# Attention and two feed-forward layers on one core: one transfer of 70 long rows for the windows of values in place of six

## What is computed

```python
q_d = q.reshape(B, H, Sd, factor, D).mean(axis=3)        # factor = 4; k_d, v_d likewise
out_d = sm_attn(q_d, k_d, v_d)                           # softmax attention over 144 means
out_up = np.repeat(out_d, factor, axis=2)
mask = np.abs(pos[:, None] - pos[None, :]) < factor      # 7 positions wide
out_local = softmax(where(mask, scale * q @ k.T, -1e9)) @ v
x = (out_up + out_local).transpose(0, 2, 1, 3).reshape(B * S, H * D)     # 2304 x 512
x = elu(x @ w_in0) @ w_out0                              # 512 -> 2048 -> 512
out = (s * relu(x @ w_in1) ** 2 + b) @ w_out1
```

## Time and profile before

| | us |
|---|---|
| median of 3 runs | 888.83 |
| lowest, highest | 888.66, 889.57 |
| the profiled execution | 886.9 |
| its span | 885.1 |
| PE busy in the span | 853.1 (96%) |
| DVE busy | 621.1 (70%) |
| ACT busy | 448.7 (51%) |
| POOL busy | 66.7 (8%) |

### The profile page before, as it was taken

One profiled execution on the slowest core, in us unless ns is written; L12 is line 12 of the kernel. 1 busy time (PEld: TensorE's weight loads), 2 busy tenths in 40 slices (PEclk: granted clock), 3 DMA queues, 4 the chain that ended last, 5 costly groups with the idle time before them and its releaser, 6 DMA issues.

```text
span 885.1 us, 14880 instructions
## 1 busy us (share of the span) xinstructions
PE 853.1 (96%) x5660; PEld 777.0 (88%) x5660; DVE 621.1 (70%) x976; ACT 448.7 (51%) x928; POOL 66.7 (8%) x84
## 2 busy tenths in 40 slices
PE   5999789999999999999999999999999999999997
PEld 4888789999989999999999889989889898898995
DVE  6999887787776666755658886887756558555553
ACT  7999976545655344453435543535433235332322
POOL 5556510000000000000000000000000000000000
PEclk9999999999999999999999999999999999999999
DMA  8789925645525434353352654636645344553411
GB/s 193 189 185 201 207 63 193 213 155 190 213 91 218 168 128 170 131 185 136 129 194 74 211 178 163 207 131 228 211 143 190 131 138 171 190 189 133 138 52 72
DMA packets 44192, 143.94 MB, mean 163 GB/s; under 512 B 5120, under 2 KB 15200, under 8 KB 44128
## 3 DMA queue, kind: packets, MB, share of 16 engines
q1 hardware_dynamic: 44128, 143.07, 49.7%
HBM read 108.97 MB, written 34.08 MB: 162 GB/s over the span
## 4 chain that ended last, share of the span: by engine, by line
PE 84%; DVE 5%; ACT 3%; issue 3%; POOL 2%; DMA 2%; SPq 1%; DVEq 0%; POOLq 0%; ACTq 0%
PE ps_h L600 36%; PE ps_y L636 22%; PE ps_y L629 21%; DMA qbd<-in_qt 2%; PE ps_h L549 1%; PE ps_s L472 1%; ACT prob L669 1%; POOL v L438 1%; POOL q_half L431 1%; DVE hsum L1103 1%; PE ps_xd L525 1%; PE ps_t L496 1%; DVE prob L923 1%; DVE xs_lo L974 1%; PE ps_sd L481 1%
## 5 line engine op out<-in xcount | busy, mean ns | idle before, releaser
L1103 DVE TENSOR_TENSOR hsum<-hsum,ps_h 128x384 f32<-128x384 f32 x322 | 176.9, 551 | 167.0 <-PE ps_h L600 164.3
L600 PE MATMUL ps_h<-xs_hi,wc_hi 128*128 128x384 f32 x644 | 218.8, 340 | 1.8 <-DVE hsum L1103 1.6
L600 PE MATMUL ps_h<-xs_lo,wc_hi 128*128 128x384 f32 x644 | 217.4, 338 | 0.0
L600 PE MATMUL ps_h<-xs_hi,wc_lo 128*128 128x384 f32 x644 | 217.3, 337 | 0.0
L820 ACT ACTIVATE act_out<-act_out,sb 128x768 f32<-128x768 f32 x48 | 49.5, 1031 | 228.6 <-DVE act_out L1118 228.6
L600 PEld LDWEIGHTS ps_h<-xs_hi,wc_hi 128*128 128x128 f32 x644 | 121.0, 188 | 12.2 <-issue 1.5
L600 PEld LDWEIGHTS ps_h<-xs_lo,wc_hi 128*128 128x128 f32 x644 | 121.0, 188 | 8.8
L1124 DVE TENSOR_TENSOR g_lo<-act_out,g_hi 128x768 fp32r<-128x768 f32 x96 | 91.5, 954 | 49.6 <-ACT g_hi L831 49.6
L600 PEld LDWEIGHTS ps_h<-xs_hi,wc_lo 128*128 128x128 f32 x644 | 121.0, 188 | 0.0
L636 PE MATMUL ps_y<-wo_hi,g_hi 128*128 128x512 f32 x288 | 113.0, 392 | 1.5 <-ACT xsum L841 1.5
L636 PE MATMUL ps_y<-wo_hi,g_lo 128*128 128x512 f32 x288 | 113.9, 395 | 0.0
(11 more groups left out here) (89 smaller groups left out, 1089.7 us busy)
## 6 DMA issues: line engine op xcount, KB each, us to landing
wc_hi<-wc_kept SPq DMA_DIRECT2D x30, 896.0 KB, 4.5
wc_lo<-wc_kept SPq DMA_DIRECT2D x30, 896.0 KB, 6.4
wstage<-in_w_out SPq DMA_DIRECT2D x48, 512.0 KB, 3.6
wc_kept<-wc_hi SPq DMA_DIRECT2D x16, 896.0 KB, 3.6
wc_kept<-wc_lo SPq DMA_DIRECT2D x16, 896.0 KB, 6.3
wstage<-in_w_in SPq DMA_DIRECT2D x18, 512.0 KB, 7.1
kall<-in_kt SPq DMA_DIRECT2D x16, 288.0 KB, 4.5
qbd<-in_qt SPq DMA_DIRECT2D x32, 144.0 KB, 4.4
```

Source lines behind the costliest of these rows:

```text
L600: mm = pe.matmul(o, wc[a][:, sl % 2, W_SLOT[k], c * P:(c + 1) * P], xs[x][:, X_SLOT[k], c, :], start=(c == 0 and q == 0), stop=(c == 1 and ...
L1103: dve.tensor_tensor(part(sl, *out_at), part(sl, *in_at), ps_h[:, prod_number(sl, pos) % 2, 0:TH], op).then_inc(h_added, 1)
```

## The change

The host lays out the values a second time: for each pair 70 rows, and in row r the r-th position of all nine windows side by side, 9 x 128 numbers, 4608 bytes. `load_v` fills `vwin` with one DMA of those 70 rows. `v4` is loaded as before from the old layout. With two DMAs for each pair, NV is 2 in place of 7.

```diff
-def attention_moe_moe2(nc, q_t, k_t, v, w_in0, w_out0, w_in1, w_out1, s, b, out):
+def attention_moe_moe2(nc, q_t, k_t, v, v_t, w_in0, w_out0, w_in1, w_out1, s, b, out):
...
-    NV = 7
+    NV = 2
...
             def load_v(bb, slot):
                 vp = v[bb, slot]
-                inner = vp[QT - REACH:QT - REACH + (NT - 2) * QT].rearrange("(t r) x -> r t x", r=QT)
-                rest = vp[2 * QT - REACH:2 * QT - REACH + (NT - 2) * QT].rearrange("(t r) x -> r t x", r=QT)
-                dst = vwin[:, slot].rearrange("p t h d -> p t (h d)")
-                sp.dma_start(dst[0:QT, 1:NT - 1, :], inner).then_inc(v_loaded[slot], 16)
-                sp.dma_start(dst[QT:WIN, 1:NT - 1, :], rest[0:2 * REACH]).then_inc(v_loaded[slot], 16)
-                for t in (0, NT - 1):
-                    a = WSTART[t]
-                    sp.dma_start(dst[0:QT, t, :], vp[a:a + QT]).then_inc(v_loaded[slot], 16)
-                    sp.dma_start(dst[QT:WIN, t, :], vp[a + QT:a + WIN]).then_inc(v_loaded[slot], 16)
+                sp.dma_start(vwin[:, slot].rearrange("p t h d -> p (t h d)"), v_t[bb, slot]).then_inc(v_loaded[slot], 16)
                 sp.dma_start(v4[:, slot].rearrange("p k i x -> p k (i x)"),
                              vp.rearrange("(k p i) x -> p k (i x)", k=2, i=POOL)
                              ).then_inc(v_loaded[slot], 16)
...
+    def lay_v_tiles(x):
+
+        tiles = [x[:, :, a:a + 70] for a in [min(max(t * 64 - 3, 0), x.shape[2] - 70) for t in range(x.shape[2] // 64)]]
+        y = np.stack(tiles, axis=3)
+        return np.ascontiguousarray(y).reshape(*y.shape[:3], -1)
...
-        "in_v": np.ascontiguousarray(v.reshape(v.shape[0], v.shape[1] // 2, 2, *v.shape[2:]).transpose(0, 1, 3, 2, 4)).reshape(
-            v.shape[0], v.shape[1] // 2, v.shape[2], 2 * v.shape[3]),
+        "in_v": pairs_of_v,
+        "in_v_tiles": lay_v_tiles(pairs_of_v),
```

More of the change, by code:

```diff
@@ L1229, in lay_w_out @@
         return np.ascontiguousarray(x.transpose(2, 0, 1, 3)).reshape(128, w.shape[0] // 256, 2 * w.shape[1])
+    def lay_v_tiles(x):
+        tiles = [x[:, :, a:a + 70] for a in [min(max(t * 64 - 3, 0), x.shape[2] - 70) for t in range(x.shape[2] // 64)]]
+        y = np.stack(tiles, axis=3)
+        return np.ascontiguousarray(y).reshape(*y.shape[:3], -1)
     nc = bacc.Bacc("TRN2", target_bir_lowering=False, num_devices=1)
+    pairs_of_v = np.ascontiguousarray(v.reshape(v.shape[0], v.shape[1] // 2, 2, *v.shape[2:]).transpose(0, 1, 3, 2, 4)).reshape(
+        v.shape[0], v.shape[1] // 2, v.shape[2], 2 * v.shape[3])
     arrays = {
```

## The result

| | before | after |
|---|---|---|
| median of 9 runs each, us | 889.57 | 894.61 |
| lowest, highest | 886.87, 891.56 | 887.08, 896.70 |
| the profiled execution, us | 886.9 | 891.17 |
| its span | 885.1 | 889.4 |

The ratio is 1.0044, with a 95% interval of 1.0026 to 1.0063: slower by 5 us in the median, where I had forecast no difference that can be told and a time of 888.4 in a range that ended at 889.8. (The two medians alone give 1.0057.) The executions scatter more than before, and the fastest of them, 887.08 us, lies inside the range of the forecast. Something happens in most executions, not in all.

The account below looks back on a forecast made before the run. PE fills 84% of the chain; the change could act only in the attention stage, through SP's late issue and the DMA backlog delaying POOL twice. The sum, -0.41 us, took the median 888.83 to 888.4, range 886.7 to 889.8.

Parts of the forecast that it names:

- (1): SP's queue: 3.29 us of issue go, one of 0.4 comes; a step falls from 5.27 to 2.4 us, SP waits for values.
- (3): POOL at pair 14, attention stage: without the wait for q's DMA it starts 0.27 us earlier, and PE and ACT follow.
- (4): POOL at pair 15: starts 1.32 us earlier, but PE gains only 0.59 and ACT keeps 0.41 us.
- (6): Pace in the loop: POOL's first addition takes 1.15 us at any DMA share, so less traffic gains zero.
- D: Rival: POOL's late starts come from the backlog of weights, k and q alone and stay; 888.8 us, chance 0.10.
- (2): DMA engines: same bytes in 70 longer rows; a pair costs 4.8 to 7.0 us now and no more afterwards.
- C: Rival, much faster: short rows disturb compute or the fetching of code, so pairs speed up; 2.8 us, 886.0, chance 0.08.
- B: Rival, slower: seventy rows spread badly, SP queues everything, DMA sets the pace; pair 15's q 3.3 us later, 892.1, chance 0.08.

## Why the prediction was wrong

**Right.** Point (1) in its mechanics: 0.33 to 0.37 us for the new issue (I took 0.4), 2.4 us for a step, SP waiting for values, pair 15's q issued at 77.7 us (I said about 79). Points (3) and (4) for POOL: its late starts on a DMA went. Point (6): 1.15 us for the addition, as before. D falls with these. Whether (4)'s 0.41 us are there can't be told; the kernel held back, which has the short issue of (1), POOL in time as in (3) and (4), and no standing queue, lies at 0.9989 and 1.0009.

**The step that failed** is in (1) and (2): "Nothing of this is on the path by itself, it only makes (1) safe". I had the capacity of the DMA engines between 172 and 251 GB/s and leaned on the upper end, from a share of 0.76 at 191 GB/s; my own 4.8 to 7.0 us for a pair reached past the 6.1 us of compute, and I wrote "under or about". But a share counts the time of packets, and this grows with the queue: 200 GB/s came at 0.93 with SP ahead and at 0.76 with it held. Kept full, the engines of the three profiles of the changed kernel gave 186 to 217 GB/s in the stretches of 12 us between 28 and 88 us, and 192 to 196 with short rows. A pair is 1.207 MB, so some 6.0 us at 200 GB/s, against 6.1 us of compute: next to nothing left to drain what the head had piled up. So my forecast for the profile, k landing near 4 us, was wrong by 10 us; the share from 76 to 100 us did fall, but only to 0.93 and 0.96; and PE's first big product, forecast at 112.3 us, came at 116.16. I had priced what SP's lateness costs (POOL's two starts) and not what it gave: a queue that drained between steps. The six short issues were a brake, 3.29 us long in each step.

**What was missing** is a third reader of the DMA engines. I asked of POOL alone what it waits for, and left out PE's code, which nobody waits for by a semaphore. It stood in the page, 42 packets of q8, and a look at when these came against the places in the unrolled steps where PE needs them would have shown margins of 4 to 6 us. C had "the fetching of code" in it, with the sign turned round.

**B** had the sign right and the mechanism wrong. It put the price into q coming late because 70 rows spread badly. In the three profiles of the changed kernel q was never late after the head, and with 630 short rows the loss is the same (1.0054 against 1.0065). Late q from full engines did show in two kernels that run ahead with the long rows, in the profile with three batches in the loop and in one held in the unrolled steps alone, so B's full engines were right, and how much of the loss in other executions they make this way stays open. The rule of the Trainium skill that I set beside it, DMA: Bandwidth & Descriptors, "Why a DMA increments its semaphore by 16 and not by 1", may hold for the split over engines; no run here shows single engines, and it explains nothing of the loss. Two other places of that page bear on what happened. "Rules for kernel authors" advises to issue a DMA early and to wait for it late; here that was the harm, 5 us, as the engines were full. And "Queues, rings and completion order" has each engine take turns between its queues packet by packet, by which a block of code would wait for a turn and not for a deep data queue; the traces show its start 3.6 to 5 us nearer to the need, so either the turn is not so short or the request itself comes later, which stays open.

**The scatter.** Executions of one kernel differ by their clock: before, those with a mean granted clock of 0.993 or more had a median of 888.0 us, those under 0.989 had 890.1. A difference of 0.4 us in the sum is below what such falls do by chance, and my range, which took the scatter of three runs (0.9 us), was too narrow even for single executions of the kernel before, 885.12 to 891.82 us. The clock alone doesn't make the loss: at 0.988 and 0.989 the executions of the changed kernel had a median of 894.9 us (8 of them), those of the kernel before 890.6 (17), 4.3 us apart, about what the standstills add up to.

## What to carry to other kernels

Before you take issue time from a queue, ask whether its slowness spaces the transfers: where bytes for a step over the rate of the full engines come near to the step's time, a faster issuer only makes the queue longer. Count code among the readers: here the unrolled steps took a block every 6 to 9 us, no semaphore shows it, and its sign in the profile was PE stopping in the middle of a run of matmuls with "issue" as releaser. If transfers are to be merged there, hold the issue by a wait that comes one step later; here that gave back all of the 5 to 6 us.

## What the runs showed of the hardware

- A busy share of DMA engines is no measure of what is left: 200 GB/s were moved at 0.76 with SP held back and at 0.93 with a standing queue.
- A block of 16 KB on q8 took 1.1 to 1.5 us between 75 and 100 us, with a full queue or without; PE went on 1.3 to 1.6 us after its end, in seven of seven standstills of the changed kernel.
- A 12 us stretch at a share of 0.90 to 0.96 held 169 to 217 GB/s of the same long rows, depending on the execution.
- At a granted clock of 0.50, four matmuls that took 0.94 us took 1.63. PE stood still for 1.74 us without a fall of the clock behind it and for 2.27 us with one (0.60 over the next 4 us); what sets it off isn't shown.
